# Routing set between the first two ups of a tile, and TensorE fed over the passage from phase 1 to phase 2

## The reference

```python
X = fft(fft(x, axis=1), axis=2).real                 # x: 4 x 3072 x 256
xk, xr = mu_k*X + (1-mu_k)*X_prev, mu_r*X + (1-mu_r)*X_prev
v = maximum(xk @ w_k, 0)**2 @ w_v                    # d_ff 1024
x3 = sigmoid(xr @ w_r) * v                           # 12288 tokens x 256
expert = argmax(x3 @ w_gate); p = softmax gate       # 8 experts
for i in tokens: if counts[e] < 384: slot[e, counts[e]++] = x3[i]
y = maximum(slot @ w1[e], 0) @ w2[e];  out[i] = p * y of its slot, 0 if dropped
```

## Time and profile before

| | |
|---|---|
| median of 3 runs | 642.27 us |
| profiled execution | 641.74 us |
| its span, first to last instruction | 639.9 us |
| PE busy | 618.6 us (97%) |
| DVE / ACT / POOL busy | 452.6 / 320.2 / 108.6 us |
| mean granted TensorE clock | 0.990 of full |

### The profile page before, as it was taken

How to read it: one execution, slowest core, us unless ns; L and a number is a source line. 1 busy time by engine, 2 the same in 40 slices (tenths; PEclk the granted TensorE clock), 3 DMA queues, 4 the chain that set the end, 5 groups by cost and what they waited for, 6 DMA issues and landing times.

```text
span 639.9 us, 10620 instructions
## 1 busy us (share of the span) xinstructions
PE 618.6 (97%) x3470; PEld 530.1 (83%) x3470; DVE 452.6 (71%) x1018; ACT 320.2 (50%) x673; POOL 108.6 (17%) x105
## 2 busy tenths in 40 slices
PE   8989999999999999999999999999994999999996
PEld 5958888888888878887888888788783999999995
DVE  4468678977776588779887766687863777666671
ACT  1566445454536654645444545654542566555550
POOL 0530112020202011202020202020206011111111
PEclk9999999999999999999999999999996999999999
DMA  8947154341410033000000000060005545555000
GB/s 318 284 118 263 61 172 158 109 149 59 166 50 21 1 96 120 16 2 8 2 9 0 8 1 2 2 200 1 4 1 189 182 160 182 182 182 182 25 25 25
DMA packets 39597, 59.70 MB, mean 93 GB/s; under 512 B 4198, under 2 KB 31159, under 8 KB 39548
## 3 DMA queue, kind: packets, MB, share of 16 engines
q1 hardware_dynamic: 35708, 52.59, 24.9%
q0 software_dynamic: 3840, 6.52, 2.9%
HBM read 36.63 MB, written 26.91 MB: 99 GB/s over the span
## 4 chain that ended last, share of the span: by engine, by line
PE 88%; DVE 5%; ACT 3%; issue 2%; DMA 1%; POOL 0%; POOLq 0%; DVEq 0%; ACTq 0%
PE bank L291 66%; PE bank L1045 4%; PE bank L1075 4%; PE bank L991 3%; PE bank L978 3%; PE bank L1003 2%; PE bank L348 2%; PE bank L1078 2%; ACT xt L569 1%; PE bank L1360 1%; DVE square L851 1%; DVE xk_raw L753 1%; ACT xk L603 1%; ACT xt L559 1%; DVE xt L742 1%
## 5 line engine op out<-in xcount | busy, mean ns | idle before, releaser
L291 PE MATMUL bank<-k,wv 128*128 128x512 f32 x672 | 166.5, 398 | 0.0
L291 PEld LDWEIGHTS bank<-k,wv 128*128 128x128 f32 x672 | 125.7, 188 | 29.7
L291 PE MATMUL bank<-xk,wk 128*128 128x512 f32 x522 | 132.9, 401 | 0.0
L620 ACT ACTIVATE relu<-bank 128x512 f32<-128x512 f32 x116 | 67.7, 597 | 123.8 <-PE bank L291 70.6
L506 POOL DMA_INDIRECT dispatched<-rows,slot x56 | 64.1, 1144 | 382.8 <-DVE slot L834 370.0
L291 PEld LDWEIGHTS bank<-xk,wk 128*128 128x128 f32 x522 | 96.0, 188 | 21.1
L851 DVE TENSOR_TENSOR square<-relu 128x512 f32<-128x512 f32 x116 | 78.9, 691 | 47.5 <-ACT relu L620 37.4
L846 DVE TENSOR_TENSOR k<-square,k 128x512 fp32r<-128x512 f32 x115 | 79.0, 687 | 4.8 <-ACT k L615 4.8
L615 ACT ACTIVATE k<-square 128x512 fp32r<-128x512 f32 x115 | 72.0, 626 | 13.0 <-DVE square L851 13.0
L291 PE MATMUL bank<-down_w,he 128*128 128x256 f32 x576 | 70.9, 284 | 0.0
L291 PEld LDWEIGHTS bank<-down_w,he 128*128 128x128 f32 x576 | 69.6, 192 | 0.0
(11 more groups left out here) (115 smaller groups left out, 791.5 us busy)
## 6 DMA issues: line engine op xcount, KB each, us to landing
out_rows<-blank SPq DMA_DIRECT2D x16, 768.0 KB
raw_up<-in_moe_w SPq DMA_DIRECT2D x8, 1024.0 KB, 4.7
raw_down<-in_moe_w SPq DMA_DIRECT2D x8, 1024.0 KB
x_area<-in_x SPq DMA_DIRECT2D x12, 512.0 KB, 3.8
dispatched<-blank SPq DMA_DIRECT2D x1, 3276.0 KB, 19.3
got<-dispatched SPq DMA_DIRECT2D x8, 409.5 KB, 6.6
y<-in_x SPq DMA_DIRECT2D x6, 512.0 KB
first_partner<-in_x SPq DMA_DIRECT2D x2, 512.0 KB
```

The lines of the kernel that those rows point to most:

```text
L291: done = nc.tensor.matmul(bank, w, x, start=first and i == 0, stop=last and i == len(terms) - 1)
L620: nc.scalar.activation(relu[:, f % 2, :], hb[f % 2][:, :], ACT.Relu).then_inc(hb_drained, 1)
```

## The change

1. In every tile that isn't the first of its sequence, PE makes up 0, then `route_rows(n - 1)`, then up 1 (each as an ordinary product that waits for both halves of the input), ACT and DVE take the routing between `hidden`/`squares` of columns 0 and 1, and `route_counts` comes after the first three of the twelve gate matmuls. In tiles 0, 6, 12 and 18 the order of the ups and of ACT and DVE stays.
2. Placing: a running `next_slot` (expert number times 384 plus the count so far) and a constant `limit` take the place of a multiplication by the expert number. Six instructions lead to the slot numbers, before seven; one that nobody in the chain waits for is added behind them. Two instructions are added ahead of the first tile.
3. SP keeps the count of scatters in a register of its own and waits for them itself; POOL's wait and `all_routed` go.
4. After leaving phase 1, PE issues eight fp32 matmuls of 128x384 that nobody reads; the two behind `turn` go.
5. The first product of each expert takes the high half of `xe` as it comes and the low half last (`first_product`), in place of a wait for all of it.

```diff
-    ROUTE_STEPS = 15
+    ROUTE_STEPS = 14
 # SP
+                    if n > 0:
+                        sp.reg_add(sent, sent, 16 * GRP)
...
-                sp.wait_ge(all_routed, 1)
+                sp.wait_ge(scattered, sp.snap(sent, min_val=16 * GRP, max_val=16 * GRP * NTILE))
 # POOL
-                pool.wait_ge(scattered, pool.snap(sent, min_val=16 * GRP, max_val=16 * GRP * NTILE))
-                pool.sem_inc(all_routed, 1)
 # ACT, before(n); DVE has the same with squares(n, 1)
                     hidden(n, 0)
-                    hidden(n, 1)
+                    if n % TILES == 0:
+                        hidden(n, 1)
                     if n > 0:
                         route(n - 1)
+                    if n % TILES:
+                        hidden(n, 1)
 # DVE, ahead of tile 0
+                    nc.vector.tensor_scalar(next_slot[:, :], expert_no, float(cap), None, ALU.mult)
+                    nc.vector.tensor_scalar(limit[:, :], expert_no, float(cap), float(cap), ALU.mult, ALU.add)
 # DVE, route_place
-                                                 base[:, :].unsqueeze(1).to_broadcast(wide), ALU.add))
-                    step(nc.vector.tensor_scalar(over[:, :, :], pos[:, :, :], float(cap), FAR, ALU.is_ge, ALU.mult))
-                    step(nc.vector.tensor_tensor(over[:, :, :], over[:, :, :], pos[:, :, :], ALU.add))
-                    step(nc.vector.scalar_tensor_tensor(pos[:, :, :], expert_no.unsqueeze(1).to_broadcast(wide), float(cap),
-                                                        over[:, :, :], ALU.mult, ALU.add))
+                                                 next_slot[:, :].unsqueeze(1).to_broadcast(wide), ALU.add))
+                    step(nc.vector.tensor_tensor(over[:, :, :], pos[:, :, :], limit[:, :].unsqueeze(1).to_broadcast(wide), ALU.is_ge))
+                    step(nc.vector.scalar_tensor_tensor(pos[:, :, :], over[:, :, :], FAR, pos[:, :, :], ALU.mult, ALU.add))
...
                     nc.vector.tensor_copy(slot[:, :], slot_f[:, :]).then_inc(slots_ready, 1)
+                    nc.vector.tensor_tensor(next_slot[:, :], next_slot[:, :], total, ALU.add)
 # PE, before(n)
-                    first_ups(n)
-                    if n > 0:
+                    if n % TILES == 0:
+                        first_ups(n)
+                        if n > 0:
+                            route_rows(n - 1)
+                    else:
+                        pe.wait_ge(mixed, len(MIXED) * n + DH + 1)
+                        up(n, 0)
                         route_rows(n - 1)
+                        up(n, 1)
                     pe.wait_ge(mixed, len(MIXED) * (n + 1) + 1)
                     pe.wait_ge(gated, DH * (n + 1))
-                    gate_in(n, 0)
-                    gate_in(n, 1)
+                    gate_in(n, 0, 0)
                     if n > 0:
                         route_counts(n - 1)
+                    gate_in(n, 0, 1)
+                    for part in range(DH):
+                        gate_in(n, 1, part)
 # PE, end of phase 1
+                walk(pe, before, after, last)
+                keep_warm_with(8, ident, small[:, 0:3 * P])
 # PE, phase 2
+                def first_product(e, i):
+                    bank, hidden = hbe[0][:, 0:cap], slice(0, P)
+                    high, low = (w[:, :, hidden] for w in up_w[i])
+                    for h in range(DH):
+                        pe.wait_ge(xe_high, e * DH + h + 1)
+                        nc.tensor.matmul(bank, high[:, h], xe[:, i, 0, h, :], start=h == 0, stop=False)
+                        nc.tensor.matmul(bank, low[:, h], xe[:, i, 0, h, :], start=False, stop=False)
+                    for h in range(DH):
+                        pe.wait_ge(xe_ready, e * DH + h + 1)
+                        done = nc.tensor.matmul(bank, high[:, h], xe[:, i, 1, h, :], start=False, stop=h == DH - 1)
+                    done.then_inc(he_full, 1)
                 turn(0, 0, 0)
-                keep_warm_with(2, ident, small[:, 0:3 * P])
...
-                        pe.wait_ge(xe_ready, (e + 1) * DH)
                         for f in range(FT):
                             pe.wait_ge(we_ready, e * PIECES + f + 1)
                             pe.wait_ge(he_ready, e * FT + max(f + 1, 3))
+                            if f == 0:
+                                first_product(e, i)
+                                continue
```

More of the change, by code:

```diff
@@ L184, in build @@
     base = ph("base", [P, EXPERTS])
+    next_slot = ph("next_slot", [P, EXPERTS])
+    limit = ph("limit", [P, EXPERTS])
     token = ph("token", [P, GRP])
@@ L257, in build @@
     rows_in = [sem("rows_in_even"), sem("rows_in_odd")]
-    all_routed = sem("all_routed")
     up0_in = sem("up0_in")
@@ L432, in _ @@
                 sp.reg_mov(loads, 32)
+                sent = sp.alloc_register("sent_sp")
+                sp.reg_mov(sent, 0)
                 load_weights()
@@ L459, in after @@
                         place_edge(n // TILES + 1)
-                walk(sp, before, after, lambda: None)
+                walk(sp, before, after, lambda: sp.reg_add(sent, sent, 16 * GRP))
                 for c in range(len(CHUNKS)):
@@ L494, in _ @@
                 pool.wait_ge(slots_blank, 16)
-                sent = pool.alloc_register("sent_pool")
-                pool.reg_mov(sent, 0)
                 def route(m):
@@ L511, in route @@
                         ).then_inc(scattered, 16)
-                    pool.reg_add(sent, sent, 16 * GRP)
                 def before(n):
@@ L875, in before @@
                     squares(n, 0)
-                    squares(n, 1)
+                    if n % TILES == 0:
+                        squares(n, 1)
                     if n > 0:
                         route(n - 1)
+                    if n % TILES:
+                        squares(n, 1)
                     squares(n, 2)
@@ L1080, in first_ups, with gate_in @@
                                 done.then_inc(hb_full, 1)
-                def gate_in(n, h):
+                def gate_in(n, h, kh):
                     cut = slice(h * P, (h + 1) * P)
-                    product(pe, rb[h][:, :], [(wr[:, 0, kh, cut], wr[:, 1, kh, cut], xr[:, 0, kh, :], xr[:, 1, kh, :]) for kh in range(DH)]
-                            ).then_inc(r_full, 1)
+                    done = product(pe, rb[h][:, :], [(wr[:, 0, kh, cut], wr[:, 1, kh, cut], xr[:, 0, kh, :], xr[:, 1, kh, :])],
+                                   first=kh == 0, last=kh == DH - 1)
+                    if kh == DH - 1:
+                        done.then_inc(r_full, 1)
                 def down(n, f):
@@ L1175, in _, with last @@
                 first_dft()
-                walk(pe, before, after, lambda: route(NTILE - 1))
+                def last():
+                    route(NTILE - 1)
+                    pe.wait_ge(routed, NTILE + 2)
+                walk(pe, before, after, last)
+                keep_warm_with(8, ident, small[:, 0:3 * P])
         phase1.close()
```

## The result

The changed kernel takes **649.04 us** (648.74 to 652.52, six runs) where the kernel before, run beside it, takes 642.33 (641.33 to 643.34): a ratio of 1.0114, 95% interval 1.009 to 1.0137. It is slower by 6.7 us and outside the predicted range, which ended at 643.6. The profiled execution took 648.74, its span is 646.9 where that of before is 639.9.

What follows compares the result with a forecast made beforehand. PE bounds the kernel (busy 618.6 of 639.9 us), and the passage between the phases is what there is to win. 1.66 us won there less 0.2 in phase 1, about 1.5, gives 640.8 us from 642.27; range 637.6 to 643.6.

Steps and rivals of the forecast that it cites:

- New order in the tiles: Phase 1: in 12 tiles two waits come earlier, with no real PE wait; 0.2 us lost in all (0 to 1.5).
- two waits: Phase 1 tiles: row products need `x3` after one up; counts need the one-hot, ready at 1.80 us against PE's 2.10.
- slower in the tiles: Rival: one-hot late, PE stands 0.3 to 0.5 us in each of 12 tiles; 645.6 us, chance 0.07.
- Tile 3's hand-over: Phase 1, tile 3: DVE's `x3` ends just as PE comes to the row products; up to 0.2 us lost.
- SP's rows: Passage: SP loads the first expert's rows at 483.3, not 485.83; they land 3.0 us later, at 486.4.
- Unread matmuls: Passage: exit 1.2 us, sixteen records at full clock 5.1 us, end at 486.7; PE transposes at 487.3 against 488.87.
- The first product: Phase 2 start: in halves at full clock, product 0 ends 2.35 us after the transposes' start; PE wants product 3 at 491.7.
- What is late next: Passage: POOL's splits hold DVE at L1300 and L1303, PE waits some 3 us, product 3 starts at 494.77.
- The two rivals of the passage: DVE gets free between POOL's splits (638.5 us, chance 0.22); the clock falls a second time (643.1 us, chance 0.17).
- the second fall of the clock: Rival: PE stands 3.1 us ahead of product 3, starts it at half clock, 0.85 us slower; 643.1 us, chance 0.17.
- The forecast 1.66: Passage: product 3 at 494.77 in place of 496.43, 1.66 us won before taking off 0.2 for phase 1.
- the forecast case: Main case, DVE held by both of POOL's splits: 640.8 us, holding 639.9 to 642.5, chance 0.45.

Runs made afterwards that it cites:

- e1: Changed kernel with the counts of tiles 6 and 12 put back behind all twelve gate matmuls: 641.96 us, ratio 0.9996 to the kernel before.
- e2: Kernel before with only the counts of tiles 6 and 12 moved to after three gate matmuls: 648.17 us, ratio 1.0086.
- e3: Changed kernel with three unread matmuls ahead of the counts in tiles 6 and 12, filling PE's wait: 647.73 us, ratio 1.0087 to the kernel before.
- e8: Kernel before with parts 1 to 3 alone, counts of tiles 6 and 12 left behind the gate matmuls: 640.68 us, ratio 0.9971.
- e5: e4 with four unread matmuls at the exit in place of eight: 640.06 us, in two groups of four runs, ratio 0.9961 to the kernel before.
- e6: e4 with no unread matmuls at the exit: 641.14 us, ratio 0.9977 to the kernel before.
- e11: e9 with DVE telling PE that the weights are ready ahead of its low halves: 638.46 us, ratio 0.9939 to the kernel before.
- e10: e9 with the first product of each expert whole, as before the change: 638.96 us, ratio 0.9948 to the kernel before.
- e4: e1 with DVE's gate weights made after hidden block 4, not ahead of block 0: 639.88 us, ratio 0.9954 to the kernel before.
- e9: e5 with two more unread matmuls ahead of the transposes and one behind them: 638.56 us, ratio 0.9936 to the kernel before.

## Why the prediction was wrong

**The step that failed** is "New order in the tiles", at its first sentence: "It applies to 12 of the tiles run (1 to 5, 7 to 11, 13, 14)". That is true of the row products and of ACT's and DVE's order, but not of the second of the "two waits" that "come earlier": the counts moved ahead of nine gate matmuls in tiles 6 and 12 too, while ACT and DVE kept the old order there. The diff shows it: `route_counts` stands under `n > 0`, the rest under `n % TILES`. Point 1 of "The change" reads as if the counts moved only in the tiles with the new order, and is wrong in the same way. I weighed PE's 2.10 us against a one-hot at 1.80 for the twelve, and costed nothing for the two. Their cost was to be read from the timeline of before, at tile 6:

```profile
231.48 3.06 PE L291 MATMUL bank<-xr,wr 128*128 128x512 f32 x12
...
234.33 0.19 DVE L809 TENSOR_TENSOR padded<-score,toprank 128x32 bf16<-128x32 f32 x1
...
234.57 0.10 PEld L1052 LDWEIGHTS bank<-padded,earlier 128*128 128x128 bf16 x1 [0.46 <-DVE padded L809]
```

Three of the twelve end about 0.9 us behind 231.48, at 232.4, and the counts can't load before 234.57: PE stands 2.1 us. e1 takes the placement out and e2 sets it alone into the kernel before.

**The clock behind that wait** I could not have put at a number. The only fall in before came 2.9 us after PE stopped, and I took less as safe. It fell behind 2.14 and 2.15 us in after, and held behind 2.14 in one tile of e2. The two steps of the table make 2 × 3.64 = 7.3; with them the forecast 640.8 would have been 648.1, against 649.04. Of the rest, 0.5 is there before tile 1, and 0.5 is the passage, which gained less than forecast (below).

**The rival "slower in the tiles"** had the mechanism, PE waiting for the one-hot, and a time (645.6) for the wrong place: 0.3 to 0.5 us in twelve tiles. There it did not occur. With a chance of 0.07 it also shows that the range, drawn from cases that all took the diff's reach as read, left out the one question that decided.

**Phase 1's other terms.** No wait in the twelve tiles, as said. Tile 3's hand-over cost 0.1 us by the table (up to 0.2 allowed). But 0.5 us is there from tile 1 on. The first transform product starts at 8.74 and not at 8.09. e1 and e2 have the 0.5 as well, but e3, whose code is the same up to there, starts it at 8.16 and stands at −0.1 in tile 1. So it belongs to the single execution and to no edit. Between tiles 3 and 4 another 0.1 came, unexplained.

**SP's rows.** They were asked for 2.7 us behind the last up, forecast 483.3 − 480.37 = 2.9: right, and e8 shows that this part works by itself. The landing was taken over from before at 3.0 us; it took at least 3.7. That cost nothing here, since PE came later still (the rows at 494.9 at the earliest, the transposes at 495.99), but it is what PE waits for in e5, e6 and e8. Why it takes longer stays open.

**Unread matmuls.** 1.68 us of exit (forecast 1.2), 5.43 us for the sixteen records (5.1), clock at full throughout. The transposes came 7.5 us behind the last up, forecast 6.9: 0.6 late, and PE, not the rows, set it.

**The first product** started 1.7 us behind the transposes and ended at 499.0, 3.0 behind them where 2.35 was put down: DVE tells PE that the weights are ready only after its own two halves of `xe`, so the halves gain less than they could. e11 moves that, e10 takes the halves away, and both move the time by no more than can be told.

**What is late next** was right: DVE is held by both of POOL's splits. `L1321` ends at 500.35 and `L1324` at 502.66, and at their ends POOL's two instructions of 2.35 us each end as well (half of 4.69 from 497.94 is 500.29; the end is 502.63). The rule cited from the Trainium skill, "SBUF — State Buffer", section "Who interferes with whom", held for both lines: each took over 2.1 us and ended with one of POOL's instructions. PE's wait was 2.08 us, forecast 3.1: measured from the last up, PE came to it 12.6 us behind (forecast 11.3; the 0.6 and 0.7 above), and DVE was ready 0.3 us later than forecast. POOL started 0.7 later than forecast, and 0.4 came back because L1324 ended with POOL's instruction and not behind it. The two rivals of the passage fell: L1324 was held too, and the second fall of the clock was not seen in after. In sum the passage gained 15.9 − 14.7 = 1.2 us from the last up to product 3. The forecast 1.66 took 496.43 for product 3 in before, from the chain view, where the timeline has 496.27; with that it is 1.5, and DVE's 0.3 is the difference.

**What the sum left out.** The sum counts parts 4 and 5 as a gain. They were a loss: parts 1 to 3 alone gain 15.9 − 13.6 = 2.3 us from the last up to product 3 (e8). The prediction had seen that PE waits away what it gains ahead of POOL's end. But it had POOL start at 487.2, as in before (487.13), and did not ask where it would start without the unread matmuls: 4.4 us behind the last up in e8, where it was 6.8 in before and is 7.5 in after. A slip without weight: with the unread matmuls at 482.4 and 1.5 us lost in phase 1, the forecast case reaches 642.9 and not 642.5.

e4 and e9 show the way round: with the gates later, they are computed when POOL's splits are over (0.17 us for the `tensor_scalar`, 0.14 for the cast in e9), and the version e9 is faster than both kernels, 0.6% below before and 1.6% below the changed one.

## What to carry to other kernels

When a step is moved by a line that isn't under the same condition as the moves that make room for it, list for each instance (each tile, each first tile of a sequence) what stands ahead of the wait and what ends it; two instances out of fourteen cost 7 us here, where the passage won 1.2. A wait of about 2 us on PE is to be priced twice, once for itself and once, with a chance, for the half-speed stretch behind it. And before a passage is tightened for one engine, find the work of the next engine that will be in its way, and move that first: the same move was worth nothing before and 2.1 us after. Where work is added to keep an engine busy ahead of a barrier, count what the barrier lets start on the other engines: eight unread matmuls moved POOL's start by 3.1 us, and with parts 4 and 5 the kernel was 1.3 us slower than without them.

## What the runs showed of the hardware that was not expected

- **The clock falls behind shorter gaps than before showed, and not always.** It fell behind waits of 2.14 and 2.15 us in after, behind one of two equal ones in e2 (tile 6, 2.14 us, held; tile 12, 2.15, fell), and behind exits of 2.00 us in e3 and 2.02 in e4, where PE had been at work again for about 1.2 us when it fell; behind 1.98 in e1 and 1.97 in e9 it held in the profiled runs. In e5 an exit of 1.80 us and two gaps of 1.77 and 0.88 us with six transposes between preceded it. Four of e5's eight runs are 3 us slower than the other four and have the lower mean clocks (0.991 to 0.994 against 0.995 to 0.999), which fits a fall in some executions only; but only one was traced.
- **A tiny DVE operation can take as long as POOL's instruction.** 128 x 3 elements, 0.17 and 0.14 us by the earlier trace rows, took 2.11 and 2.18 us, a `tensor_scalar` and a cast, the latter with a strided source. It is not every operation: the reciprocal of 128 x 3 elements between them ran from 500.39 to 500.57, inside POOL's second instruction (500.3 to 502.6), in its usual 0.18 us.
- **The time between two phases isn't the same for each engine and run.** PE's exit took 1.68 us in after, 1.76 in e10 and 1.8 to 2.02 in e1, e3, e4, e5, e9 and e11, in equal code. I can't say why.
- **The same load of rows doesn't take the same time to land.** The first landing took 3.0 us in before and 3.7 to 4.0 in e5, e6, e8 and e9, with an equal number of bytes. No run parts the causes.
